# One tile of a three-tile Fourier sum folded into its own rows: one matmul in place of three passes

## The reference, cut to what matters

```python
def phi(x):                                   # attention features, per head
    proj = x @ w_phi
    proj = proj - max(abs(proj), axis=-1)
    return concat([exp(proj), exp(-proj)])
num = phi(q) @ (phi(k).T @ v);  den = phi(q) @ sum(phi(k)) + 1e-6
x = num / den                                 # -> [4 batches, 576 tokens, 512 features]

X = fft(fft(x, axis=tokens), axis=features)   # the Fourier part
u = x + real(X)
u = u + relu(norm(u) @ w_ch1) @ w_ch2         # first channel MLP, 2048 hidden
u = u + (relu(u.T @ w_tok1) @ w_tok2).T       # token MLP
out = u + relu(u @ w2_ch1) @ w2_ch2           # second channel MLP, 1536 hidden
```

## Time and profile before

| | us |
|---|---|
| median of 3 runs | 975.48 (974.63 to 975.66) |
| the profiled execution, its own time | 974.76 |
| its span in the trace | 973.0 |
| TensorE matmul busy | 960.5 (99%) |
| TensorE weight load busy | 866.1 (89%) |
| VectorE busy | 478.7 (49%) |
| ScalarE busy | 311.4 (32%) |
| GpSimd busy | 184.1 (19%) |

### The profile page before, as it was taken

One profiled execution on the slowest core, in us unless ns is written; L12 is line 12 of the kernel. 1 busy time (PEld: TensorE's weight loads), 2 busy tenths in 40 slices (PEclk: granted clock), 3 DMA queues, 4 the chain that ended last, 5 costly groups with the idle time before them and its releaser, 6 DMA issues.

```text
span 973.0 us, 17986 instructions
## 1 busy us (share of the span) xinstructions
PE 960.5 (99%) x7563; PEld 866.1 (89%) x7563; DVE 478.7 (49%) x956; ACT 311.4 (32%) x605; POOL 184.1 (19%) x161
## 2 busy tenths in 40 slices
PE   8999999999999999999999999999999999999998
PEld 6989999888899989999899999877999899999997
DVE  6998888952621321322312313355684544645543
ACT  6865757544311111111111112244432212212211
POOL 3653555379700000000000000036100000000000
PEclk9999999999999999999999999999999999999999
DMA  7241333336310020010010020478220020200101
GB/s 235 78 116 42 91 113 80 113 120 200 115 65 1 1 65 1 1 65 0 0 65 0 32 82 25 141 267 313 104 87 1 1 87 1 86 2 1 44 1 44
DMA packets 50023, 70.15 MB, mean 72 GB/s; under 512 B 22944, under 2 KB 23968, under 8 KB 49824
## 3 DMA queue, kind: packets, MB, share of 16 engines
q1 hardware_dynamic: 48224, 62.83, 19.9%
q10 hardware_dynamic: 1728, 6.29, 1.7%
HBM read 50.24 MB, written 18.87 MB: 71 GB/s over the span
## 4 chain that ended last, share of the span: by engine, by line
PE 78%; DVE 2%; issue 0%; POOL 0%; ACT 0%; DVEq 0%
PE mlp_y L1088 7%; PE mlp_y L1089 7%; PE mlp_y L1087 7%; PE mlp_hid L1075 7%; PE mlp_hid L1073 7%; PE mlp_hid L1074 7%; PE mlp_y L1528 5%; PE mlp_y L1529 5%; PE mlp_y L1530 5%; PE mlp_hid L1515 2%; PE mlp_hid L1517 2%; PE mlp_hid L1516 2%; PE mlp_turn L1517 2%; PE mlp_turn L1516 2%; PE mlp_turn L1515 2%; PE tok_y L1879 1%
## 5 line engine op out<-in xcount | busy, mean ns | idle before, releaser
L1206 DVE SCALAR_TENSOR_TENSOR mlp_h_lo<-mlp_hid,mlp_h_hi 128x384 fp32r<-128x384 f32 x96 | 53.5, 557 | 250.2 <-ACT mlp_h_hi L1123 250.2
L1123 ACT ACTIVATE mlp_h_hi<-mlp_hid 128x384 fp32r<-128x384 f32 x96 | 47.2, 492 | 287.1 <-PE mlp_hid L1075 287.1
L1073 PE MATMUL mlp_hid<-mlp_ut_hi,mlp_w_hi 128*128 128x384 f32 x384 | 130.7, 340 | 0.0
L1075 PE MATMUL mlp_hid<-mlp_ut_hi,mlp_w_lo 128*128 128x384 f32 x384 | 129.4, 337 | 0.0
L1074 PE MATMUL mlp_hid<-mlp_ut_lo,mlp_w_hi 128*128 128x384 f32 x384 | 128.8, 336 | 0.0
L1087 PE MATMUL mlp_y<-mlp_w_hi,mlp_h_hi 128*128 128x512 f32 x288 | 112.7, 391 | 1.9 <-DVE mlp_h_lo L1206 1.9
L1089 PE MATMUL mlp_y<-mlp_w_hi,mlp_h_lo 128*128 128x512 f32 x288 | 113.9, 396 | 0.0
L1088 PE MATMUL mlp_y<-mlp_w_lo,mlp_h_hi 128*128 128x512 f32 x288 | 113.6, 395 | 0.0
L1449 POOL TENSOR_TENSOR mlp_w_lo<-mlp_w_raw,mlp_w_hi 128x1024 fp32r<-128x1024 f32 x12 | 28.4, 2397 | 392.6 <-DVE tok_x_lo L1937 382.1
L1528 PE MATMUL mlp_y<-mlp_w_hi,mlp_h_hi 128*128 128x512 f32 x216 | 84.5, 391 | 0.2 <-DVE mlp_h_lo L1723 0.2
L1529 PE MATMUL mlp_y<-mlp_w_lo,mlp_h_hi 128*128 128x512 f32 x216 | 84.4, 391 | 0.0
(11 more groups left out here) (209 smaller groups left out, 2142.5 us busy)
## 6 DMA issues: line engine op xcount, KB each, us to landing
mlp_w_raw<-in_w_mlp SPq DMA_DIRECT2D x14, 512.0 KB, 4.5
mlp_w_raw<-in_w_mlp ACTq DMA_DIRECT2D x12, 512.0 KB, 6.1
v<-in_v SPq DMA_DIRECT2D x16, 320.0 KB, 3.7
qk<-in_kT SPq DMA_DIRECT2D x16, 288.0 KB, 4.2
mlp_u<-u_scratch SPq DMA_DIRECT2D x6, 768.0 KB, 4.7
qk<-in_qT SPq DMA_DIRECT2D x15, 288.0 KB, 4.1
u_scratch<-x_all SPq DMA_DIRECT2D x4, 1024.0 KB, 4.7
mlp_u<-u_scratch SPq DMA_DIRECT2D x4, 1024.0 KB, 5.3
```

Of the source, the lines that this page charges most:

```text
L1073: nc.tensor.matmul(out, w_hi[:, j, col], hi, start=(c == 0), stop=False)
L1075: last = nc.tensor.matmul(out, w_lo[:, nf - 1 - j, col], hi, start=False, stop=(c == DC - 1))
L1123: nc.scalar.activation(h_hi[:, j % 2, :], hid[j % 2][:, 0:BT], ACT.Relu).then_inc(h_rounded, 1)
L1206: nc.vector.scalar_tensor_tensor(out=h_lo[:, j % 2, :], in0=hid[j % 2][:, 0:BT], scalar=0.0, in1=h_hi[:, j % 2, :], op0=ALU.max, op1=ALU.s ...
```

## The change

The third tile has only 32 rows of data in 128. The new kernel puts into the same 128 rows: the high part (rows 0 to 31), the high part again (32 to 63) and the low part (64 to 95); the table's third tile holds the matching high, low, high parts of its values. One matmul over these rows gives what three passes gave. The single token 288 takes rows 96 and 97 (high and low part), with the table's value negated, since VectorE makes these rows as (rounded times 0 or 1) minus value.

What is added for it, for each batch: `act_third` (two ScalarE casts of 32 partitions x 516 elements), `dve_third` (one VectorE subtraction of the same size), `copy_edge` (a DMA of 1 x 257 elements from one row to the next, issued by SyncE), `act_edge` (a ScalarE cast of 2 x 258) and `dve_edge` (one VectorE instruction of 2 x 258), a semaphore `third_split` that TensorE waits for before the last matmul of chunk 0, and waits on it before the next batch's folds. `act_fold` and `dve_low` shrink from three tiles to two (774 to 516 elements), and `act_fold` of the sums no longer waits for the edge row. Once per program there are a small memset on VectorE and two small copies on GpSimd (`table_hi` rows from `table_lo`), which TensorE's wait at the end of step 3 takes in.

```diff
@@ pe_over_s @@
-        for t in range(FRONT):
+        for t in range(1, FRONT):
             col = slice(base + step * t, base + step * t + n)
-            last = passes(out, fold_hi[:, k, t, first:first + rows], fold_lo[:, k, t, first:first + rows],
-                          table_hi[:, col], table_lo[:, col], t == 0, t == FRONT - 1)
-        last.then_inc(s_done, 1)
+            passes(out, fold_hi[:, k, t, first:first + rows], fold_lo[:, k, t, first:first + rows],
+                   table_hi[:, col], table_lo[:, col], t == 1, False)
+        if c == 0:
+            pe.wait_ge(third_split, b + 1)
+        nc.tensor.matmul(out, fold_hi[:, k, 0, first:first + rows], table_hi[:, base:base + n],
+                         start=False, stop=True).then_inc(s_done, 1)
@@ sync and its helper @@
+    def copy_edge(sp, b):
+        sp.wait_ge(edge_made, 2 * b + 2)
+        sp.dma_start(folds[EDGE + 1:EDGE + 2, 0, 0, 0:257], edge[:, 0:257]).then_inc(edge_copied, 16)
...
             load_v(sp, Pair(n))
+            if n % 4 == 2 and n >= 6:
+                copy_edge(sp, n // 4 - 1)
...
         mlp1["load_block"](sp, 1)
+        copy_edge(sp, LAST)
         mlp1["load_weights"](sp, 4, [0, 1])
@@ ScalarE @@
-            act.wait_ge(edge_made, 2 * b + 2)
...
-        nc.scalar.copy(fold_hi[:, k], folds[:, k, :, 0:FREQ]).then_inc(fold_rounded, 1)
+        nc.scalar.copy(fold_hi[:, k, 1:FRONT], folds[:, k, 1:FRONT, 0:FREQ]).then_inc(fold_rounded, 1)
+    def act_third(act, b):
+        for rows in GROUP[0:2]:
+            last = nc.scalar.copy(fold_hi[rows, :, 0, :], folds[GROUP[0], :, 0, 0:FREQ])
+        last.then_inc(third_rounded, 1)
+    def act_edge(act, b):
+        if b == 0:
+            act.wait_ge(third_cleared, 1)
+        act.wait_ge(edge_copied, 16 * b + 16)
+        nc.scalar.copy(fold_hi[edges, 0, 0, :], folds[edges, 0, 0, 0:FREQ]).then_inc(edge_rounded, 1)
@@ VectorE @@
+    def dve_third(dve, b):
+        dve.wait_ge(third_rounded, b + 1)
+        nc.vector.tensor_tensor(fold_hi[GROUP[2], :, 0, :], folds[GROUP[0], :, 0, 0:FREQ], fold_hi[GROUP[0], :, 0, :],
+                                ALU.subtract)
+    def dve_edge(dve, b):
+        dve.wait_ge(edge_rounded, b + 1)
+        nc.vector.scalar_tensor_tensor(out=fold_hi[edges, 0, 0, :], in0=fold_hi[edges, 0, 0, :],
+                                       scalar=ident_a[edges, EDGE + 1:EDGE + 2], in1=folds[edges, 0, 0, 0:FREQ],
+                                       op0=ALU.mult, op1=ALU.subtract).then_inc(third_split, 1)
@@ dve_step @@
                     dve_low(dve, k // 4 - 1, 1)
+                    dve_third(dve, k // 4 - 1)
                 dve_norm(dve, Pair(k - 1))
+                if k % 4 == 1 and 5 <= k:
+                    dve_edge(dve, k // 4 - 1)
@@ the last batch, scalar_beside and vector_beside, j == 0 @@
             act_fold(act, LAST, 1)
+            act_third(act, LAST)
+            act_edge(act, LAST)
             mlp1["act_weights"](act, [2])
...
             dve_low(dve, LAST, 1)
+            dve_third(dve, LAST)
+            dve_edge(dve, LAST)
```

More of the change, by code:

```diff
@@ L109, in front @@
     fold_s, fold_d = folds[:, 0], folds[:, 1]
-    edge = folds[ROWS[2]:ROWS[2] + 1, 0, 0]
+    GROUP = [slice(ROWS[2] * n, ROWS[2] * n + ROWS[2]) for n in range(3)]
+    EDGE = 3 * ROWS[2]
+    edge = folds[EDGE:EDGE + 1, 0, 0]
+    edges = slice(EDGE, EDGE + 2)
     qk = at("qk", [128, 2, 2 * S], F32, 158720)
@@ L173, in front @@
     edge_made = sem("edge_made")
+    edge_copied = sem("edge_copied")
+    edge_rounded = sem("edge_rounded")
+    third_cleared = sem("third_cleared")
+    third_rounded = sem("third_rounded")
+    third_split = sem("third_split")
     odd_folded = sem("odd_folded")
@@ L454, in tensor @@
             if k == 3:
-                pe.wait_ge(table_split, 3)
+                pe.wait_ge(table_split, 5)
     def tensor_beside(pe, what, j):
@@ L556, in act_step @@
                 act_fold(act, k // 4 - 1, 1)
+                act_third(act, k // 4 - 1)
+            if s == 3 and k % 4 == 1 and 5 <= k:
+                act_edge(act, k // 4 - 1)
             if s == 2:
@@ L666, in dve_sum @@
             dve.wait_ge(fold_split, 2 * b - 1)
+            dve.wait_ge(third_split, b)
         x = x_of(b)
@@ L697, in dve_low @@
         dve.wait_ge(fold_rounded, 2 * b + k + 1)
-        nc.vector.tensor_tensor(fold_lo[:, k], folds[:, k, :, 0:FREQ], fold_hi[:, k], ALU.subtract).then_inc(fold_split, 1)
+        nc.vector.tensor_tensor(fold_lo[:, k, 1:FRONT], folds[:, k, 1:FRONT, 0:FREQ], fold_hi[:, k, 1:FRONT],
+                                ALU.subtract).then_inc(fold_split, 1)
+    def dve_third(dve, b):
[7 more added lines that the diff above has]
+                                       op0=ALU.mult, op1=ALU.subtract).then_inc(third_split, 1)
     def dve_piece(dve, b, i):
@@ L750, in vector @@
         nc.vector.memset(ab_hi[:, 2, :].bitcast(F32), 0.0).then_inc(ab_cleared, 1)
+        nc.vector.memset(fold_hi[EDGE:128, :, 0, :].bitcast(F32), 0.0).then_inc(third_cleared, 1)
         for half in ek:
@@ L795, in pool_fold @@
             pool.wait_ge(fold_split, 2 * b)
+            pool.wait_ge(third_split, b)
         x = x_of(b)
@@ L858, in pool_step @@
             pool.wait_ge(table_split, 3)
+            for n, cols in enumerate((slice(TC, TC + SFREQ), slice(TS, TS + HALF))):
+                nc.gpsimd.tensor_copy(table_hi[GROUP[1], cols], table_lo[GROUP[1], cols]).then_inc(table_split, 1)
+                pool.wait_ge(table_split, 4 + n)
             for tile in (0, 5):
@@ L2124, in constants @@
     table[0, first:first + HALF + 1] = (ks % 2 == 0)
-    table[ROWS[2], TC:TC + HALF + 1] = (ks % 2 == 1)
+    for base, step in ((TC, SFREQ), (TS, HALF)):
+        for n in range(1, 3):
+            table[ROWS[2] * n:ROWS[2] * n + ROWS[2], base:base + step] = table[0:ROWS[2], base:base + step]
+    table[3 * ROWS[2]:3 * ROWS[2] + 2, TC:TC + HALF + 1] = -(ks % 2 == 1).astype(np.float64)
     d = np.arange(D // 2).reshape(2, 128)
```

## The result

| | before | after |
|---|---|---|
| median of 15 runs each | 975.17 (974.63 to 975.90) | 977.80 (976.62 to 980.09) |
| ratio, after to before | | 1.0027 [1.0019, 1.0035] |
| profiled execution, own time | 974.76 | 976.62 |
| its span | 973.0 | 974.5 |

The forecast was 975.3 in a range of 973.2 to 977.5. The interval begins just under the 0.2% that can be told from no change: the kernel is slower.

The account below looks back on a forecast made before the run. TensorE, 99% busy, was taken to wait for VectorE at the end of step 5. Terms: -1.06 + 0.06 + 0.80 = -0.2 us on 974.76, 974.6; from the median 975.3, range 973.2 to 977.5, no difference forecast.

Parts of the forecast that it names:

- Once per program: Memset on VectorE and two GpSimd copies in step 2: taken as 0; without cover 0.9 to 2 us once.
- Batches 0 and 1: End of steps 5 and 9: TensorE 0.55 late, chunks 1 to 4 give back 0.27 each; -0.53 per batch.
- The bound's reason: End of step 5: TensorE up to 0.9 late if the edge's wait on ScalarE and the start add 0.35.
- the rival of the cheap edge: Edge cheap, nothing waits for it: batches 0 and 1 give 0.8 to 1.33 each; -2.0 to -3.0 in all; chance 0.16.
- Batch 2: Third batch, to 190.01: VectorE has no wait for TensorE; gaps before ScalarE's casts absorb most of +0.28, leaving +0.06.
- The last batch: ScalarE's longer queue delays GpSimd's low part by 1.1, so TensorE starts the fourth weight chunk +0.8 us later.
- The late copy: Last batch: the edge row's copy lands after 208.2 and ScalarE's queue waits for it; 977.1 to 978.1, chance 0.14.
- The port rival: Last batch: VectorE and GpSimd hinder each other reading SBUF; chain 0.4 later, sum +0.2, 975.7; chance 0.10.
- the step 3 term: End of step 3: offset between the kernels predicted as 0.
- the 255 us term: In the MLP, near 255 us: offset predicted as 0; no row of the prediction touched this place.

Follow-up runs that it names:

- e1: Kernel before plus only two GpSimd copies of the same size as the change's, in step 2: 975.78, ratio 1.0009.
- e3: Changed kernel with its GpSimd table copies a step later and token 288's row left out (no copy, cast or edge instruction): 974.53, ratio 0.9999.
- e8: Changed kernel with its GpSimd table copies a step later and the third tile's subtraction on GpSimd instead of VectorE: 978.32, ratio 1.0042.
- e9: Changed kernel with table copies a step later and, in the last batch, ScalarE's weight chunk cast ahead of the fold casts: 981.29, ratio 1.007.
- e10: Same as e9, but token 288's row by its high part alone: one ScalarE cast, no copy, no edge instruction: 977.70, ratio 1.0027.
- e4: Changed kernel with table copies a step later and VectorE's low part of the differences moved from before the norm to step 6: 980.03, ratio 1.0056.

## Why the prediction was wrong

- **Once per program, "I take nothing": wrong, +0.80.** The prediction looked for who waits for the copies' result. Nobody does; what counted is what they pushed: GpSimd's next run, into a VectorE instruction on the path (e1).
- **Batches 0 and 1, -0.53 each: the mechanism right, the size wrong.** TensorE was 1.04 late at `num`, where 0.55 was forecast and 0.9 was the upper bound, and got 1.03 back of a forecast 1.08. On VectorE the stall was 0.90, not 0.46. The edge instruction was taken as 0.38 and is 0.62 (e3: 0.61). The bound's reason, a wait on ScalarE, did not come: its cast ended at 69.86, 1.66 before. Without the edge, as in e3, a batch wins 0.78, which is what the rival of the cheap edge gave it (0.8 to 1.33). The shorter low parts and the third one cost 0.29, not 0.09: three instructions take 2.03 and not 1.83.
- **Batch 2, +0.06: wrong, +0.52.** It was hoped that early casts would take up the stall; with a stall of 0.90 in place of 0.46 on VectorE they take up 0.38, and the rest, 0.52, stays, since VectorE ends the wait of the earlier trace rows.
- **The last batch, +0.80: the chain right, the size +1.30.** GpSimd starts 1.45 later and not 1.1. ScalarE's last cast ends 0.26 later than forecast (211.03 less 1.27 is 209.76, not 209.5), and GpSimd starts 0.14 behind it, not 0.05. And the slack of 0.34 at the fourth chunk was only 0.19: TensorE starts 0.15 after GpSimd's end even when it waits (225.38 to 225.53). 1.45 - 0.19 = 1.26. The late copy, the rival for "slower", did not happen.
- **The port rival** was put at +0.4, at one place, with a chance of 0.10. There it took another form: GpSimd's fold had its 1.00, VectorE's `fold_lo` beside it was held (1.54 in place of 0.69), and nobody waited for that, since the chain went through ScalarE. The same mechanism set the step 3 term and, with the other sign, the 255 us term, so it moved about 1.8 us of the ledger, at places that the prediction did not look at. The Trainium skill (SBUF — State Buffer, "SBUF: two separate sides") has it as an exclusive lock: the one that starts first keeps the pair for its whole instruction, and the other blocks. By that rule step 3 and e8 agree. So do e9 and e10: there VectorE got in when GpSimd's one subtraction of 2.34 ended, though GpSimd had its next instruction right behind. The 255 us rows go further: VectorE arrived at 252.31, in the third of GpSimd's five instructions of 2.37 each, and got in only when all five were over (6.46); after, it was passed over once. In e4 it was passed over three times (4.22). The measurement decides: the hold can last beyond one instruction, and when it does is open.
- **Near 255 us, 0: wrong, -1.05,** a wait of the kernel before that the prediction had not read, since the change touches nothing there.

The sum of the misses, 0.80 + 1.05 + 0.46 + 0.50 - 1.05 = 1.76, is the way from -0.2 to 1.56. So the steps that failed are the copies taken at nothing, the edge instruction taken at 0.38, and a wait near 255 us not read at all. The medians are 1.07 further apart than the ledger (2.63). Of that, 0.3 lies outside the span of the two profiled executions; the cause of the rest stays open.

## What to carry to other kernels

Forty matmuls fewer were worth nothing, because each batch paid for them with two instructions on the queue that TensorE was already waiting for: price an instruction there by the distance from its predecessor's end to the next start (0.62, not 0.38). And when an edit moves GpSimd by a microsecond, look beside its run for VectorE instructions that read SBUF, small ones too (128 x 2 elements were held for 6.46): they can be held to the end of GpSimd's instruction or beyond, and a relief on one engine (e4, e8, e9) can turn into a longer hold on the other.

## What the runs showed of the hardware

- VectorE held beside GpSimd: 1.66 for 0.56 (381 elements), 4.22 for 0.56, 2.57 for 0.69 (32 partitions), and 6.46 and 3.89 for an instruction of 128 x 2 elements. Each ended 0.03 to 0.6 us behind the end of a GpSimd instruction, and the last one at the end of the fifth or of the fourth of five, by when it had come.
- A GpSimd instruction that starts beside a VectorE one grows too: 1.39 for 1.00, 3.13 for 2.81 for the two of `qk_lo`. The weight subtraction, which was there first, did not: 2.34 beside VectorE and 2.39 without.
- A transfer of one row of 257 elements, SBUF to SBUF, issued at 206.62, was not late for a reader at 209.56.
- The same subtraction of 32 x 516 took 1.58 on GpSimd in place of 0.69 on VectorE; its first 0.53 lay beside a VectorE instruction, and no run has it alone.
